# One recurrent chunk of a fused mLSTM and MLP kernel is summed by feature instead of by token

## The reference

```python
for t in range(S):
    m_new = np.maximum(f_gate[:, :, t] + m, i_gate[:, :, t])
    f_stab = np.exp(f_gate[:, :, t] + m - m_new)
    i_stab = np.exp(i_gate[:, :, t] - m_new)
    C = f_stab * C + i_stab * outer(v_t, k_t)
    n = f_stab * n + i_stab * k_t
    nq = sum(n * q_t)
    y[:, :, t] = sigmoid(o_gate) * (C @ q_t) / max(|nq|, 1)
x = y as (1536, 320)
h = x @ w_in                          # 320 -> 2048
x = (h - tanh(h)) @ w_out             # 2048 -> 320
p = domain_probs / sum
out = sum over 4 experts of p[:, e] * (relu(x @ w1[e]) @ w2[e])   # 320 -> 1024 -> 320
```

## Time and profile before

| | |
|---|---|
| time, median of 3 runs | 586.46 us (586.42 to 586.52) |
| the profiled execution | 586.45 us, span 584.7 us |
| PE busy | 580.0 us (99%) |
| DVE, ACT, POOL busy | 224.7, 200.6, 126.3 us |
| granted TensorE clock | full over the whole span |
| DMA | 43.83 MB, mean 75 GB/s |

### The profile page before, as it was taken

The page is one execution under the profiler, slowest core; times in us unless marked ns, Lnnn a source line. Parts: engine busy times, 40 slices in busy tenths (PEclk is TensorE's granted clock), DMA queues, the critical chain, the costliest instruction groups (busy, mean ns, idle before and its releaser), DMA issues.

```text
span 584.7 us, 8954 instructions
## 1 busy us (share of the span) xinstructions
PE 580.0 (99%) x3662; PEld 529.5 (91%) x3662; DVE 224.7 (38%) x451; ACT 200.6 (34%) x398; POOL 126.3 (22%) x99
## 2 busy tenths in 40 slices
PE   8999999999999999999999999999999999999997
PEld 7999999999998888899999999999999999999997
DVE  6667655565555333423131313131313232322222
ACT  5775645565544555511123211123211111111111
POOL 4968322233200444400004400004300000000000
PEclk9999999999999999999999999999999999999999
DMA  7987545654220132300003300001000000001011
GB/s 285 327 280 284 201 133 167 169 165 100 52 39 1 53 100 100 114 32 1 0 1 99 100 1 0 1 1 49 2 1 1 1 1 0 1 0 46 1 45 46
DMA packets 35342, 43.83 MB, mean 75 GB/s; under 512 B 18670, under 2 KB 27878, under 8 KB 35302
## 3 DMA queue, kind: packets, MB, share of 16 engines
q1 hardware_dynamic: 35302, 43.26, 23.2%
HBM read 38.85 MB, written 4.40 MB: 74 GB/s over the span
## 4 chain that ended last, share of the span: by engine, by line
PE 99%; DVE 0%; issue 0%; ACT 0%; DVEq 0%
PE bank L1212 11%; PE bank L1211 11%; PE bank L1213 11%; PE bank L1267 10%; PE bank L1266 10%; PE bank L1265 9%; PE bank L1215 6%; PE bank L1214 6%; PE bank L1237 5%; PE bank L1238 4%; PE bank L1239 4%; PE bank L1032 2%; PE bank L1245 2%; PE bank L1246 2%; PE bank L1046 2%; PE bank L1075 1%
## 5 line engine op out<-in xcount | busy, mean ns | idle before, releaser
L1009 DVE SCALAR_TENSOR_TENSOR g_lo<-bank,g_hi 128x512 fp32r<-128x512 f32 x96 | 66.4, 691 | 253.4 <-ACT g_hi L732 253.4
L732 ACT ACTIVATE g_hi<-bank 128x512 fp32r<-128x512 f32 x96 | 57.5, 599 | 269.8 <-PE bank L1215 269.7
L1267 PE MATMUL bank<-w_all,g_lo 128*128 128x320 f32 x384 | 118.7, 309 | 0.0
L1266 PE MATMUL bank<-w_all,g_hi 128*128 128x320 f32 x384 | 118.5, 309 | 0.0
L1212 PE MATMUL bank<-x_lo,w_all 128*128 128x512 f32 (+2 forms) x318 | 118.2, 372 | 0.0
L1265 PE MATMUL bank<-w_all,g_hi 128*128 128x320 f32 x384 | 118.2, 308 | 0.0
L1211 PE MATMUL bank<-x_hi,w_all 128*128 128x512 f32 (+2 forms) x318 | 118.0, 371 | 0.0
L1213 PE MATMUL bank<-x_hi,w_all 128*128 128x512 f32 (+2 forms) x318 | 117.0, 368 | 0.0
L518 POOL TENSOR_TENSOR w_all<-w_raw,w_all 128x1408 fp32r<-128x1408 f32 x16 | 51.7, 3233 | 192.5 <-ACT w_all L609 192.5
L1265 PEld LDWEIGHTS bank<-w_all,g_hi 128*128 128x128 f32 x384 | 72.1, 188 | 3.7
L1266 PEld LDWEIGHTS bank<-w_all,g_hi 128*128 128x128 f32 x384 | 72.1, 188 | 3.7
(11 more groups left out here) (148 smaller groups left out, 648.0 us busy)
## 6 DMA issues: line engine op xcount, KB each, us to landing
w_raw<-in_w SPq DMA_DIRECT2D x24, 704.0 KB, 4.2
feat<-in_feat SPq DMA_DIRECT2D x12, 512.0 KB, 4.8
tok<-in_tok SPq DMA_DIRECT2D x12, 484.0 KB, 5.8
zb<-z SPq DMA_DIRECT2D x10, 512.0 KB, 4.7
out<-arena SPq DMA_DIRECT2D x12, 160.0 KB, 1.9
spare<-xg SPq DMA_DIRECT2D x7, 256.0 KB, 2.8
fb<-f SPq DMA_DIRECT2D x14, 80.0 KB
xg<-feat SPq DMA_DIRECT2D x14, 80.0 KB
```

The lines of the kernel that those rows point to most:

```text
L732: A(g_hi[:, b, 0:N], h_ps[b][:, 0:N], ACT.Relu).then_inc(ghi_ready, 1)
L1009: V.scalar_tensor_tensor(g_lo[:, b, 0:N], h_ps[b][:, 0:N], 0.0, g_hi[:, b, 0:N].bitcast(F32), ALU.max, ALU.subtract).then_inc(g_ready, 1)
L1266: mm(out, g_hi[:, b, t], low_w, start=False, stop=False)
L1267: last = mm(out, g_lo[:, b, t], high_w, start=False, stop=stop)
```

## The change

Chunk 2 is summed by feature as chunks 5 to 11 are; chunks 3 and 4 stay by token. Its factors are made at k = 5 (step 8) and its high and low parts at k = 10 (step 13), where chunk 2 was turned in step 7 and had its parts there. Counts in waits now come from how many chunks of each form came before (`ord_feat`, `ord_tok`, `ord_x`). The rows of chunks 3 and 4 go into `tok` instead of `yt`, since `xg` lies over `yt`. GpSimd gets `scale_q(2)`, `decay_state(2)` and `gate_x(2)` between the splits of the pieces. SP's queue up to the loads of chunk 7 is written anew.

```diff
-FACTORS, FEAT_TURN = 4, 8
+FACTORS = {n: 5 if n == 2 else 4 for n in range(2, STEPS)}
+FEAT_TURN = {n: 10 if n == 2 else 8 for n in range(2, STEPS)}
...
+def by_feature(n):
+    return n == 2 or n >= FEAT
+def ord_feat(n):
+    return len([k for k in range(n + 1) if by_feature(k)])
+def ord_tok(n):
+    return len([k for k in range(n + 1) if not by_feature(k)])
+def ord_x(n):
+    return {2: 4, 3: 3}.get(n, n + 1)
...
+        def y_of(n):
+            return yt[:, n, :] if n < BATCH else tok[:, n % RING, 0:D]
...
             load_z(2)
-            load_tok(2)
-            load_z(3)
-            sp.dma_start(probs[:, :, :], probs_d).then_inc(probs_in, 16)
-            sp.wait_ge(p_done, 2 * BATCH)
-            load_feat(2)
-            load_piece(3)
-            load_piece(4)
-            sp.wait_ge(weigh_done, 2)
-            sp.dma_start(f_d, weigh[:, 1, :]).then_inc(f_out, 16)
-            behind = {3: (5, 6), 4: (7,), 5: (8,), 6: (9,), 7: (10,)}
-            for n in range(RING, FEAT + RING):
-                sp.wait_ge(sums_ready, n - RING + 1)
-                load_feat(n)
-                sp.wait_ge(y_ready, n - RING + 1)
-                load_tok(n)
-                if n <= FEAT:
-                    sp.wait_ge(exp_done, 2 * n)
-                    load_z(n + 1)
-                if n == RING:
-                    sp.wait_ge(f_out, 16)
-                if n == FEAT:
-                    load_f(n)
-                for k in behind.get(n, ()):
-                    load_piece(k)
...
+            sp.wait_ge(weigh_done, 2)
+            sp.dma_start(f_d, weigh[:, 1, :]).then_inc(f_out, 16)
+            load_tok(2)
+            sp.wait_ge(p_done, 2 * BATCH)
+            load_feat(2)
+            load_z(3)
+            sp.dma_start(probs[:, :, :], probs_d).then_inc(probs_in, 16)
+            sp.wait_ge(f_out, 16)
+            sp.wait_ge(fb_clear, 1)
+            load_f(2)
+            load_piece(3)
+            for n in (3, 4):
+                sp.wait_ge(sums_ready, n - RING + 1)
+                sp.wait_ge(y_ready, ord_tok(n - RING))
+                load_feat(n)
+                load_tok(n)
+                if n == 3:
+                    load_piece(4)
+            sp.wait_ge(exp_done, 6)
+            load_z(4)
+            load_piece(5)
+            sums_by_token(2)
+            load_piece(6)
+            sp.wait_ge(exp_done, 8)
+            load_z(5)
+            factors_by_feature(2)
+            load_piece(7)
+            sp.wait_ge(rows_out_d, 32)
+            load_feat(5)
+            load_tok(5)
+            sp.wait_ge(q_scaled, 1)
+            load_f(5)
+            load_piece(8)
+            sp.wait_ge(exp_done, 10)
+            load_z(6)
+            for n in (6, 7):
+                sp.wait_ge(sums_ready, n - RING + 1)
+                load_feat(n)
+                sp.wait_ge(t_ready, ord_tok(n - RING))
+                load_tok(n)
+                load_piece(n + 3)
...
             weigh_v(2)
+            scale_q(2)
             cut_z(3)
+            decay_state(2)
             split_low(3)
             split_low(4)
             weigh_v(3)
             cut_z(4)
             split_low(5)
             split_low(6)
+            gate_x(2)
             weigh_v(4)
...
-                        if k == SUMS + 1 and n < FEAT:
+                        if k == SUMS + 1 and not by_feature(n):
                             gate_rows(n, c_ps)
...
-                        if k == FACTORS and n >= FEAT:
+                        if k == FACTORS[n] and by_feature(n):
                             factors(n)
                             if n < STEPS - 1:
                                 turn_factors(n)
```

More of the change, by code:

```diff
@@ L449, in _ @@
                 if n + 1 < STEPS:
-                    sp.wait_ge(q_scaled, n - FEAT + 1)
+                    sp.wait_ge(q_scaled, ord_feat(n))
                     load_f(n + 1)
@@ L708, in _ @@
                     for n, k in phase(m):
-                        if turns(n, k) and n < FEAT:
+                        if turns(n, k) and not by_feature(n):
                             x_high(n, c_ps)
-                        if turns(n, k) and FEAT <= n < STEPS - 1:
+                        if turns(n, k) and by_feature(n) and n < STEPS - 1:
                             x_high_feat(n)
@@ L979, in _ @@
                         if turns(n, k) and n < STEPS - 1:
[L980 removed]
+                            x_low(n, xg[:, :, 0, :] if by_feature(n) else by_row(c_ps))
                         if k == 1:
                             scores(n, 0, a_ps)
[L983 removed]
+                        if k == SUMS + 1 and not by_feature(n):
                             gate_rows(n, c_ps)
[L985 removed]
+                        if k == FACTORS[n] + 1 and n == STEPS - 1:
                             turn_factors(n)
@@ L992, in _ @@
                             scores(n, 1, b_ps)
-                        if k == SUMS and n < FEAT:
+                        if k == SUMS and not by_feature(n):
                             finish_sums(n)
-                        if k == FACTORS and n >= FEAT:
+                        if k == FACTORS[n] and by_feature(n):
                             factors(n)
@@ L1058, in inter_feat @@
             def inter_feat(n):
-                pe.wait_ge(q_scaled, n - FEAT + 1)
+                pe.wait_ge(q_scaled, ord_feat(n))
                 for pair in range(PAIRS):
@@ L1165, in attention @@
                     scores(n, (a_ps, b_ps))
-                if k == SUMS and n < FEAT:
-                    pe.wait_ge(xlo_done, n)
+                if k == SUMS and not by_feature(n):
+                    if by_feature(n - 1):
+                        pe.wait_ge(sums_out, ord_feat(n - 1))
+                    else:
+                        pe.wait_ge(xlo_done, ord_x(n - 1))
                     pe.wait_ge(state_ready, n)
@@ L1171, in attention @@
                     new_state(n, b_ps, 0)
-                if k == SUMS and n >= FEAT:
-                    pe.wait_ge(xlo_done, FEAT)
-                    after(pe, sums_out, n - FEAT)
+                if k == SUMS and by_feature(n):
+                    if by_feature(n - 1):
+                        pe.wait_ge(sums_out, ord_feat(n - 1))
+                    else:
+                        pe.wait_ge(xlo_done, ord_x(n - 1))
                     pe.wait_ge(state_ready, n)
@@ L1178, in attention @@
                     new_state(n, b_ps, 0)
-                if k == TURN and n < FEAT:
+                if k == TURN and not by_feature(n):
                     turn(n, c_ps)
```

59 lines of the change are left out of this document (31 added, 28 removed).

## The result

The changed kernel takes 588.59 us (median of 16 executions, 587.49 to 591.4), the kernel before 586.53 (16 executions beside them); the ratio is 1.0041, interval 1.003 to 1.0051. It is slower, by twice the 0.2% that I called measurable, where I had forecast 587.3 and no change. The profiled execution took 588.83 us, span 586.8.

A forecast was written before the change was run, and what follows sets the result against it. PE was taken as the bound, busy 99% of the span, so every wait costs its length. Terms -1.32 + 0.48 + 0.15 + 0.92 + 0.56 = +0.79 us gave 587.24, with up(8)'s possible tenth 587.3; range 585.5 to 588.7.

The forecast's parts named there:

- Gain: Chunk 2's sums in step 5 get shorter (-0.89 us) and its turn in step 7 goes (-0.43): -1.32 us together.
- A: Step 6, GpSimd: chunk 2's state decay ahead of piece 3's split makes PE wait before up(6), +0.48 us.
- C: Step 8, VectorE: chunk 2's factors ahead of chunk 3's second scores make PE wait inside intra(3), +0.92 us.
- D: Step 13, VectorE: chunk 2's low parts ahead of chunk 4's gated rows make PE wait before down(13), +0.56 us.
- B: Step 7: the gating chain, no longer covered by chunk 2's turn, makes PE wait before down(6), +0.15 us.
- Rival 6: Matmul columns set the price: a loss of 0.4 us instead of the gain, 589.0 us; chance 0.02.
- possibly a tenth: Up(8) meeting piece 4's split: 0, at most 0.2 us; a possible tenth raised 587.24 to 587.3.
- rival 5: ACT is held by a piece (3 or 7) beyond its slack: 588 to 589 us; chance 0.05.
- rival 4: Chunk 2's denominators land late, delaying its factors in step 8: PE waits 1.4 us more, 588.7, or half, 588.0; chance 0.20.
- same: Outcome not told from no change, within about 0.2%: 585.29 to 587.63 us; chance 0.56.
- "faster" by a full gain: Rival 3: the gain in full, PE's waits nil or half of A only, 585.1 to 585.3 us; chance 0.09.

The follow-up runs named there:

- the version without A, C and D: Changed kernel with chunk 3's second scores ahead of chunk 2's factors, chunk 2's low parts later in step 13, piece 3's split before chunk 2's decay: 585.87 us.
- the last pair of versions: Changed kernel with scores first and chunk 2's low parts later, without and with piece 3's split ahead of chunk 2's decay: 586.14 and 585.87 us.
- the kernel before held: Kernel before the change, with only four scratch fills on VectorE in step 8 ahead of chunk 3's second scores: 588.63 us.
- the B edit: Changed kernel with piece 4's load issued directly behind piece 3's, ahead of chunk 3's feat and tok: 589.86 us.
- the products in the wait: Changed kernel with six unread matrix products on TensorE between the halves of chunk 3's masked products: 588.48 us.
- the D edit: Changed kernel with chunk 2's high and low parts made in step 12 instead of step 13: 588.54 us.
- With GpSimd quiet: The C edit, plus GpSimd's weighing for chunk 5 and cut of chunk 6's gate moved behind its scaling and decay of chunk 5: 586.57 us.
- the version with the low parts behind: The C edit, plus chunk 2's low parts made behind step 13's hidden layer's low parts and chunk 4's state: 586.14 us.
- the A, B and D edits: The A one: changed kernel with GpSimd's split of piece 3 ahead of its decay of chunk 2's state, 589.33 us; B and D have their own lines.
- the C edit: Changed kernel with chunk 3's second scores ahead of chunk 2's factors on VectorE in step 8: 586.97 us.

## Why the prediction was wrong

**Gain, -1.32: right.** The rows of chunk 5 carried over exactly (2.28 us), and the version without A, C and D stands at -1.14 at up(8), the gain with B's 0.22 (1.32 - 0.22 = 1.10). Rival 6, that columns set the price, is out: 24 passes of 128 columns and the 16 small ones of `new_state` took 2.28 us where the old form took 3.17.

**A, +0.48: right**, 0.47. (By its own numbers the prediction's term is 0.51: the split's end, 32.67, and 0.15 are 32.82.) The decay began at 30.11 (forecast 30.10), the split of piece 3 at 30.80 (30.85), up(6) at 32.69 (32.80). Undone, it gives 0.43 back at up(6), and in the last pair of versions 0.27 of it reached the end.

**B, +0.15 and "possibly a tenth": right as a term**, 0.21 or 0.22 in nine traces. In the changed kernel's profiled execution it is 0.69, since piece 4 landed at 33.4, 1.6 us later than in any other. Of this the prediction had the mechanism, as rival 5, for pieces 3 and 7, with 0.05; it was piece 4 and in that execution alone of ten.

**C, +0.92: right in mechanism and place**, 0.80 in this trace, 0.69 from the kernel before held in the same place. Of rival 4, the denominators landing late: they landed at 39.6 to 41.4 in ten traces (forecast 39.7, bounds 38.8 to 40.6), and in three of them VectorE waited for them: 0.12 us in the B edit (landed 40.4), 0.46 with the products in the wait (41.2), 0.61 in the D edit (41.4). The last two traces stand 0.5 us later from before up(0) on, VectorE with them. So it happens, in part of the executions, and the price is about half of what the rival gave.

**What failed, first: D, +0.56, in size and in place.** The step is "It adds 0.77 (61.02 to 61.79 for chunk 4's)". Chunk 4's low parts read a PSUM bank; chunk 2's read SBUF, beside a GpSimd that works. They took 1.63 us, and D is 1.38. With GpSimd quiet they take 0.71 and D is 0.46. The order quoted ahead of the prediction names the new source, and the prediction priced it from the other. The place failed too, at "The turn of chunk 4 is 0.4 later too, but under the same wait": the turn is what PE waits for. And 1.38 is the D of four traces, not of every execution: the spans of the five fastest leave 0.6 to 0.8 for it.

A row of such a hold stood in the trace of before, two microseconds ahead of the rows of D. VectorE's decay of the state, with two SBUF sources, took 0.49 us twice and 0.83 in step 13, beside GpSimd, and ended 0.36 behind GpSimd's L526:

```profile
46.59 0.49 DVE L860 TENSOR_TENSOR state<-state,arena 104x328 f32<-104x328 f32 x1
57.42 0.83 DVE L860 TENSOR_TENSOR state<-state,arena 104x328 f32<-104x328 f32 x1
57.15 0.74 POOL L526 TENSOR_TENSOR arena<-tok,wa 128x328 f32<-128x328 f32 x1
```

The Trainium skill says this ("SBUF — State Buffer", Who interferes with whom): a VectorE instruction with two SBUF inputs contends with a GpSimd instruction that reads SBUF, the ports that they share are an exclusive lock, and the order of issue decides which of the two blocks. The ten traces of the changed kernel and its variants agree. Beside a working GpSimd, the 41 low-part instructions with a PSUM source never took more than 0.42 and 0.30 us, while the 36 with an SBUF source took up to 1.14 and 1.81; the 124 with an SBUF source and no GpSimd beside them took at most 0.43 and 0.29. An L948 that began 0.23 us ahead of GpSimd's L574 (59.29 and 59.52, in the version with the low parts behind) took 0.29. With this rule and the times of the changed kernel's trace, D comes out, as an estimate, at 0.56 plus the remainder of L574 behind L948's start, 0.94 us (60.80 less 59.86): 1.5 in all, for the 1.38 measured.

**What failed, second: a wait costs its own length, and nothing more.** That stood in the first paragraph. C's wait of some 0.6 us is followed in part of the executions by 3.41 us at half clock: with that wait in the kernel, 22 of 40 executions have a mean clock of 0.997 or less (7 of 16 of the changed kernel, 4 of 4, 3 of 4, 4 of 9 in the A, B and D edits, 4 of 7 of the kernel before held), and without it none of 51 of the variants. With the wait filled by work it was none of 6. Where the clock holds, the changed kernel takes 587.49 to 588.83, median 587.63, which is a third of a us above the forecast and at the edge of my "same". The five fastest have in their spans just the forecast's sum (+0.8 to +1.0, forecast +0.79), and their third of a us is the 0.2 to 0.3 outside the span, a term that the prediction hasn't got. The 7 executions with the low clock take 2.1 to 3.8 us more than this median. They, and the four in which the clock holds and the span is 586.2 or more, lift the median of all to 588.59. It takes both: with the clock held in all of them, or with the four as fast as the five, the median would be about 587.6. That the wait in step 9 sets it off is shown by the two opposite experiments: put into the kernel before by itself it brings the fall in 4 of 7 (none in the 18 beside them), and filled it brings none. Why an equal wait does so in half of the executions, and why none of the traces has such a stretch behind the 1.2 us wait in step 13 (the executions at 0.994 may have two) or behind the 1.3 us wait of the C edit's trace, stays open.

Of the range's chances: "faster" by a full gain was not there, and rivals 4 and 5 together, 0.25 for slower, were half right in kind. That 588.59 lies within 585.5 to 588.7 is luck: the upper end was set for denominators that come late, and not for the held instructions and the clock that took the time there. The signs of the terms were right. What the sum lacked is D's 0.82 in part of the executions, two to almost four us by the clock in 7 of 16, and 0.2 to 0.3 outside the span.

## What to carry to other kernels

When an instruction moves to other data, price it by a row with the same kinds of sources: VectorE with two SBUF sources beside GpSimd is another instruction than VectorE with one PSUM source, and moving it by one step only exchanges which GpSimd instruction holds it. On an engine that never waits, the first half-microsecond wait may cost more than its length, so look at the clock of every execution, not only of the profiled one. Three of the four waits went by putting first, on the engine that was waited for, what TensorE needs first.

## What I had not expected of the hardware

- VectorE's L948 (64x128) took 0.29 us alone and 0.73, 1.08 and 1.81 beside GpSimd; it ended 0.14 to 0.15 us behind the GpSimd instruction.
- A wait of 0.50 us of TensorE, in a stretch otherwise full, was followed by the half clock (1.2 GHz) about two us later, for 3.41 us in the one trace of this kernel. 4 of its 7 executions have the mean clock of this one, 0.997, and took about 1.8 us more than the other three.
- A load of 704 KB in the same place of the queue landed 9.2 to 10.5 us after its issue in seven traces, and 11.6 in one; the 4 KB of denominators took 2.5 to 4.3.
